# Attention and two MLPs in one kernel: value blocks as long rows, other orders for the first weights, turns ahead of local scores

## What is computed

```python
q_d = q.reshape(B, H, Sd, 4, D).mean(axis=3)          # the same for k_d, v_d; Sd = 144
out_up = np.repeat(sm_attn(q_d, k_d, v_d), 4, axis=2)
mask = np.abs(pos[:, None] - pos[None, :]) < 4
scores = np.where(mask, scale * np.matmul(q, k.transpose(0, 1, 3, 2)), -1e9)
attn = softmax(scores)
x = (out_up + np.matmul(attn, v))                      # as (2304 tokens, 512)
h = x @ w_in;  x = (h - np.tanh(h)) @ w_out            # d_ff 2048
gate = 1.0 / (1.0 + np.exp(-(x @ w_gate)))
out = (gate * (x @ w_val)) @ w_out2                    # d_ff 1536
```

## Time and profile before

| | us |
|---|---|
| median of 3 runs (lowest, highest) | 932.12 (931.35, 934.47) |
| profiled execution, its own time | 935.37 |
| span of the profile | 933.6 |
| mean granted clock of TensorE | 0.982 |

### The profile page before, as it was taken

The page is one execution under the profiler, slowest core; times in us unless marked ns, Lnnn a source line. Parts: engine busy times, 40 slices in busy tenths (PEclk is TensorE's granted clock), DMA queues, the critical chain, the costliest instruction groups (busy, mean ns, idle before and its releaser), DMA issues.

```text
span 933.6 us, 15654 instructions
## 1 busy us (share of the span) xinstructions
PE 894.9 (96%) x6056; PEld 837.6 (90%) x6056; DVE 588.9 (63%) x919; ACT 387.2 (41%) x752; POOL 294.0 (31%) x237
## 2 busy tenths in 40 slices
PE   7889987999999999999998999999999999999997
PEld 4666786999999999999997999999999999999996
DVE  7778884757865657765668556566544456544444
ACT  5667953435432325332343644454222233222221
POOL 5789946773103000020016565722200001000000
PEclk9798998999999999999999999999999999999999
DMA  8989837667564545454421777769775555565511
GB/s 234 208 182 221 229 121 296 251 242 296 195 217 157 217 156 211 160 213 157 170 91 46 284 292 280 280 281 368 280 285 206 211 205 204 205 269 203 203 45 68
DMA packets 46089, 197.01 MB, mean 211 GB/s; under 512 B 3936, under 2 KB 15552, under 8 KB 33216
## 3 DMA queue, kind: packets, MB, share of 16 engines
q1 hardware_dynamic: 41984, 166.66, 51.4%
q0 software_dynamic: 4032, 29.36, 8.3%
HBM read 139.90 MB, written 56.10 MB: 210 GB/s over the span
## 4 chain that ended last, share of the span: by engine, by line
PE 83%; DMA 4%; DVE 3%; ACT 3%; POOL 3%; issue 3%; SPq 1%; ACTq 0%; DVEq 0%
PE banks L827 43%; PE banks L899 19%; PE banks L1016 16%; DMA v_win<-in_v_dram 2%; DMA win_raw<-in_moe_w_in_dram 1%; PE banks L805 1%; DVE x_op L1368 1%; PE banks L782 1%; DMA qk<-in_k_dram 1%; ACT prob_d L1058 1%; POOL win L619 1%; POOL mid L633 1%; ACT win L1080 1%; PE banks L818 1%; PE banks L760 1%
## 5 line engine op out<-in xcount | busy, mean ns | idle before, releaser
L827 PE MATMUL banks<-x_op,pair 128*128 128x384 f32 x1512 | 276.9, 335 | 1.8 <-DVE cg_sum L1545 1.8
L827 PEld LDWEIGHTS banks<-x_op,pair 128*128 128x128 f32 x1512 | 265.2, 188 | 9.7 <-DVE cg_sum L1545 2.1
L899 PE MATMUL banks<-g_parts,mid 128*128 128x384 f32 x1152 | 228.2, 337 | 12.8 <-DVE x_all L1447 6.7
L899 PEld LDWEIGHTS banks<-g_parts,mid 128*128 128x128 f32 x1152 | 203.6, 189 | 14.7 <-DVE x_all L1450 7.7
L827 PE MATMUL banks<-x_op,win 128*128 128x384 f32 x1008 | 203.7, 337 | 2.7 <-ACT x_op L1117 1.4
L827 PEld LDWEIGHTS banks<-x_op,win 128*128 128x128 f32 x1008 | 178.3, 189 | 4.0 <-ACT x_op L1117 1.9
L1016 PE MATMUL banks<-wout,p_parts 128*128 128x512 f32 x648 | 163.6, 393 | 1.7 <-issue 1.7
L1450 DVE TENSOR_TENSOR x_all<-banks,x_all 128x384 f32<-128x384 f32 x168 | 92.6, 555 | 78.2 <-PE banks L899 77.7
L1016 PEld LDWEIGHTS banks<-wout,p_parts 128*128 128x128 f32 x648 | 120.2, 188 | 22.6 <-issue 2.1
L1570 DVE TENSOR_TENSOR x_all<-banks,x_all 128x512 f32<-128x512 f32 x90 | 62.1, 690 | 113.3 <-PE banks L1016 113.3
L1138 ACT ACTIVATE banks<-c_sum 128x384 f32<-128x384 f32 x72 | 35.2, 489 | 96.9 <-DVE c_sum L1417 52.6
(11 more groups left out here) (97 smaller groups left out, 1009.0 us busy)
## 6 DMA issues: line engine op xcount, KB each, us to landing
pair<-kept_pair SPq DMA_DIRECT2D x24, 1792.0 KB, 10.8
win<-kept_in SPq DMA_DIRECT2D x16, 1792.0 KB, 7.3
kept_pair<-pair SPq DMA_DIRECT2D x12, 1792.0 KB, 12.0
mid<-kept_mid POOLq DMA_DIRECT2D x16, 1024.0 KB, 5.1
kept_in<-win SPq DMA_DIRECT2D x7, 1792.0 KB, 5.8
wout<-kept_out POOLq DMA_DIRECT2D x12, 1024.0 KB, 11.6
kept_mid<-mid SPq DMA_DIRECT2D x7, 1024.0 KB, 6.2
kept_out<-wout SPq DMA_DIRECT2D x6, 1024.0 KB, 14.9
```

What stands on the lines that cost most here:

```text
L827: mm = pe.matmul(bk[:, 0:T], weights[:, w, p - 1, kk, :], x_op[:, p - 1, x, kk, :], start=(first and kk == 0 and a == 0), stop=(last and k ...
L899: mm = pe.matmul(bk[:, 0:T], w[:, wp, f, m * P:(m + 1) * P], g[:, gp, 2 * f + t, :], start=(f == 0 and a == 0), stop=(f == 1 and a == 2))
```

## The change

1. The host writes a second copy of the values, `v_windows`, of shape (4, 4, 70, 9, 128): the 9 windows of a unit side by side, so that each of the 70 partitions of `v_win` is one contiguous row of 1152 elements, 4608 bytes. `load_v` is one DMA in place of three.
2. TensorE does the two `turn_local(t-1)` ahead of `local_scores(t+1)`.
3. Quad 2: its raw load at unit 8 (was 14), its sums in iterations 14 and 15 (were after the loop), its high part at iteration 17 (was after the copies of step 1).
4. From quad 3 on: the raw load of quad 3 stands ahead of the wait for the end of the attention; the sums on GpSimd are made one step earlier in the order (n+3, ahead of `plain_low(n+1)`), the low part after it; the high part of quad n+1 stands in step n ahead of tanh of C11 (was quad n+2, ahead of tanh of C21).
5. `x_high(0, 2)` moves from iteration 16 to the end of 15, and VectorE does `x_low(0, 4)` ahead of `second_weight_low`.

```diff
 def load_v(u):
     wait(sp, s_val, u - 1)
-    for w, n in ((0, 1), (1, NW - 2), (NW - 1, 1)):
-        src = bass.AP(unit.tensor, unit.offset + FIRST_KEY[w] * P, [[P, KW], [QW * P, n], [1, P]])
-        sp.dma_start(v_win[u % 2][:, w:w + n, :], src).then_inc(s_v[u % 2], 16)
+    sp.dma_start(v_win[u % 2][:, :, :], v_windows[u // PAIRS, u % PAIRS]).then_inc(s_v[u % 2], 16)
...
-                if u == 14:
+                if u == 8:
                     load_raw(2)
             load_raw_mid(1)
+            load_raw(3)
+            keep_win(1)
             sp.wait_ge(s_x, UNITS)
-            for n in range(N1):
-                if 3 <= n + 2 < Q1:
+            for n in range(1, N1):
+                if 4 <= n + 2 < Q1:
                     load_raw(n + 2)
                 elif Q1 <= n + 2 < N1:
                     load_win(n + 2)
-                if 1 <= n + 1 < Q1:
+                if n + 1 < Q1:
+                    load_raw_mid(n + 1)
                     keep_win(n + 1)
-                if 1 <= n < Q1:
+                if n < Q1:
                     keep_mid(n)
-                if 2 <= n + 1 < Q1:
-                    load_raw_mid(n + 1)
...
 GpSimd
-            weight_sums(2, (0, 1))
+                if t == 14:
+                    weight_sums(2, (0, 1))
+                if t == 15:
+                    weight_sums(2, (2, 3))
             x_last_sum(0)
-            weight_sums(2, (2, 3))
             weight_low(2)
             for n in range(N1):
-                if 3 <= n + 2 < Q1:
-                    weight_sums(n + 2)
-                    weight_low(n + 2)
+                if n + 3 < Q1:
+                    weight_sums(n + 3)
                 if n + 1 < Q1:
                     plain_low(n + 1)
+                if n + 3 < Q1:
+                    weight_low(n + 3)
                 if n % Q1 == 3:
                     x_sums(n // Q1 + 1)
...
 TensorE
-                if t + 1 < UNITS:
-                    local_scores(t + 1)
                 if 1 <= t <= UNITS:
                     turn_local(t - 1, 0)
                     turn_local(t - 1, 1)
                 if t + 1 < UNITS:
+                    local_scores(t + 1)
                     down_scores(t + 1)
...
 ScalarE, step n
+                if 3 <= n + 1 < Q1:
+                    weight_high(n + 1)
                 tanh(n, C11)
                 tanh(n, C22)
                 g_high(n, 0)
-                if 3 <= n + 2 < Q1:
-                    weight_high(n + 2)
 ScalarE, iteration t
                 if t == UNITS:
                     copy_c(0, C11)
-                    x_high(0, 2)
                     x_high(0, 5)
                 if t == UNITS + 1:
                     x_high(0, 4)
+                    act.wait_ge(s_vd, UNITS)
+                    weight_high(2)
                     tanh(0, C11)
...
+                if t == UNITS - 1:
+                    x_high(0, 2)
...
             copy_c(1, C21)
-            act.wait_ge(s_vd, UNITS)
-            weight_high(2)
             plain_high(1)
 VectorE, after the loop
+            x_low(0, 4)
             second_weight_low()
-            x_low(0, 4)
             add_c(0, C11)
```

More of the change, by code:

```diff
@@ L40, in attention_and_mlps @@
     v: bass.AP,
+    v_windows: bass.AP,
     w_in: bass.AP,
@@ L389, in load_v @@
             def load_v(u):
-                unit = v_flat[u * P * S:(u + 1) * P * S]
                 wait(sp, s_val, u - 1)
-                for w, n in ((0, 1), (1, NW - 2), (NW - 1, 1)):
-                    src = bass.AP(unit.tensor, unit.offset + FIRST_KEY[w] * P, [[P, KW], [QW * P, n], [1, P]])
-                    sp.dma_start(v_win[u % 2][:, w:w + n, :], src).then_inc(s_v[u % 2], 16)
+                sp.dma_start(v_win[u % 2][:, :, :], v_windows[u // PAIRS, u % PAIRS]).then_inc(s_v[u % 2], 16)
             def two_chunks(src, first, step):
@@ L798, in local_values @@
             def local_values(u):
-                pe.wait_ge(s_v[u % 2], 48 * (u // 2 + 1))
+                pe.wait_ge(s_v[u % 2], 16 * (u // 2 + 1))
                 pe.wait_ge(s_cl, 2 * (u + 1))
@@ L1642 @@
         args.append(nc.dram_tensor(f"in_{name}_dram", a.shape, _mybir.dt.from_np(a.dtype), kind="ExternalInput").ap())
+        if name == "v":
+            first = [min(max(64 * w - 3, 0), s - 70) for w in range(s // 64)]
+            a = _np.ascontiguousarray(_np.stack([a[:, :, f:f + 70, :] for f in first], axis=3))
+            arrays["in_v_windows_dram"] = a
+            args.append(nc.dram_tensor("in_v_windows_dram", a.shape, _mybir.dt.from_np(a.dtype), kind="ExternalInput").ap())
     shape = (b * s, h * d)
```

## The result

The changed kernel takes 921.84 us, the median of 4 runs (920.45 to 924.27), beside 933.3 for the kernel before in the same set (931.35 to 934.83): a ratio of 0.988, 95% interval 0.985 to 0.991. Two later sets of six gave medians of 923.25 and 921.96; over all 16 runs it is 922.0 (920.3 to 927.95). So the change gains 1.2%, where 909.0 us (904 to 920), 2.5%, was predicted. The profiled execution took 924.27 (span 922.5) against 935.37 (933.6), so 11.1 us have to be found where the sum said 23.1.

The account below looks back on a forecast made before the run. TensorE was 96% busy, with all that can move before 212 us: GpSimd's work and waits in the attention, VectorE's end, stalls in steps 2 and 5. 8.7 + 2.8 + 12.6 - 1.0 = 23.1 off 932.12 gave 909.0 us, range 904 to 920.

Parts of the forecast that it names:

- Step 1: Attention's value blocks as 4608 B rows: 3.0 us less queue time per unit, GpSimd's early waits 11.6 us shorter.
- Rival A: Short rows were no burden, so the attention's early waits stay: 920.6 us, 8%.
- Step 2: Turns ahead of local scores on TensorE in the attention: counted 0, bounds -1 and +1 us.
- Step 3: Quad 2's sums inside GpSimd's full attention loop: costs 2.9 us; its high part costs 0.
- Step 5: End of the attention, from `normalise(15)` to product 3 of step 0: 11.6 us in place of 14.4, gain 2.8.
- rival B: GpSimd's low part of quad 2 goes first and VectorE waits 4.1 us at the attention's end: 913.1 us, 20%.
- Step 4: Quads 3 on in the first MLP: TensorE's stalls in steps 2 and 5, 8.9 and 3.7 us, both go: 12.6.
- Quad 7: Its sums come late behind `x_sums(1)` in step 6: 1.0 us lost, bounds 0 and 3.7.
- Rival C: In the new order of quads 3 to 7 one stall remains or comes, priced 8.9 us: 917.9 us, 10%.
- Rival D: Turns bind VectorE to GpSimd within one attention unit, 2.9 us lost in each of 14: 950 us, 5%.

Follow-up runs that it names:

- experiment 2: Kernel before with only the host's value layout and one DMA in place of three: 933.0 us, ratio 1.001 to the kernel before.
- the bench: Loads alone, without attention and MLPs, 12 blocks of each kind: 70 partitions took 21.1 us with 512 B rows, 20.1 with 4608 B; 128 rows of 2520 B 13.2.
- experiment 5: Changed kernel with both value blocks of a unit written over 128 partitions from unit 2 on (values then wrong): 915.94 us, ratio 0.983 to the kernel before.
- experiment 4: Changed kernel with local scores put ahead of the turns again: 924.21 us, ratio 0.992 to the kernel before.
- Experiment 8: Changed kernel with quad 2's four weight sums put back behind the last attention unit: 921.6 us, ratio 0.989 to the kernel before.
- experiment 10: Kernel before with only the new order of loads, sums and splits for the late quads: 924.1 us, ratio 0.992 to the kernel before.
- experiment 6: Changed kernel with the first middle weights loaded after unit 5's value block, not unit 2's: 922.26 us, ratio 0.988 to the kernel before.
- experiment 13: Changed kernel with quad 2's sums behind the last unit and quad 7's middle weights ahead of the first reload: 921.25 us, ratio 0.991 to the kernel before.

## Why the prediction was wrong

**Step 1 failed, and makes up nearly all of the miss:** 11.6 us were counted and experiment 2 shows none, of the 12.8 between 909.0 and 921.84. It put 0.100 us on each 512 B packet because 2494 of them stood in a stretch with a full queue. The other packets there were priced at the rate of a stretch with only 128-partition transfers, and the whole rest was charged to the short ones. But the groups cover 72 partitions and were slow too, and the long rows cover 70 and stayed slow. A block went from 21.1/12 = 1.8 us to 1.7 in the bench, not from 3.9 to 0.9. The term that was mis-sized is the 0.100 us per packet: in the bench's stretch of 70 short rows, 17 us x 16 engines x 0.99 over the 6840 packets that 206 GB/s make, it is about 0.039 us. The packets under 2 KB did fall as was said, from 15552 to 5024 in the whole profile, and nothing came of it. With experiment 5 the waits did go, so what comes next, GpSimd at its own pace, was right as well. The Trainium skill states what decides, on the page "SBUF — State Buffer", section "Door 1: The DMA port swizzle (why `[64,N]` ≈ `[32,N]`)": partitions 0 to 63 reach half of the ports and 64 to 127 the other half, while a step of 32 stays on the same port. The rows agree: 64 rows at 0 (208 GB/s) as slow as 32 rows (208), and 64 rows at 32 (343) nearly as fast as 128 (365). The page that the prediction weighed, "DMA: Bandwidth & Descriptors" of the Trainium skill, section "Specifications", has 512 B as the smallest transfer for line rate; here that held to within 5 to 8% (206 against 217 GB/s over 70 partitions, 334 against 360 over 128). Rival A's premise, that short rows are no burden, thus held, at 8%, and its time, 920.6, is the nearest of all.

**Step 2** was counted as nothing; experiment 4 resolves no difference (924.21 us against 921.84 to 923.25).

**Step 3** was priced at 2.9 us; the two classes of profiles lie 62 and 65 us apart from N5 to N15, so some 3.5. With step 1 at nothing, N15 should move from 113.5 to 117; it was 109.5 to 115.0 in three executions, whose waits up to N5 differ by 6.6 us.

**Step 5** said +2.8, and N15 to F became 2.3 shorter; that the size came out right is in part luck, for step 5's own order is not what did it. Experiment 8 keeps that order, puts only the sums back behind the loop, and N15 to F is 20.1 again. The working had VectorE "no longer alternating with GpSimd" there, which is step 3's doing: the gain hangs on the sums, and what step 5 adds to it no run shows. VectorE came first, as chosen, and `second_weight_low` took 2.02, so rival B did not come; ScalarE's x_high of 4 kept VectorE waiting 4.71 us, which the working had as a series without a gap. GpSimd's low part took 5.19 us in place of 4.08; it started 1.27 us before `second_weight_low` ended, and lies off the path.

**Step 4** was right: 12.6 predicted, 12.7 measured, and shown to stand alone by experiment 10. The high part cost nothing in its gap, as said.

**Quad 7** was taken as 1.0 us lost with a bound of 3.7; it is 2.5, and by another way. The sums were in time (ScalarE's high part at 207.43 waited for nothing). What was called hidden by 1 us, `plain_low(5)` with its block behind it, was only followed to its store; behind the store in SyncE's queue stood a reload of 1.8 MB and then the middle weights.

**Rival C** is that gap, at 2.5 us and not 8.9. **Rival D** did not come: N5 to N15 grew by 3.5 us, not by ten times 2.9.

## What to carry to other kernels

Before a transfer's rows are made longer, look at which partitions it covers: blocks of 64 or 70 partitions from partition 0 got 200 to 230 GB/s with rows of 512 and of 4608 bytes alike, where 128 partitions got 330 to 365, and 64 that begin at partition 32 got 343. When a mixed, full queue is to be priced, take the prices from transfers of the same shape and not as a rest. On an engine without gaps, work moved to start earlier costs its whole length there, and the end it was moved from must gain more than that: here 3.5 us were paid for 2.3. Where a new order moves a store, follow SyncE's queue behind it to the next load that somebody waits for.

## What was not expected of the hardware

The executions of one and the same kernel differ by up to 10 us, and the mean granted clock goes with it: one kernel (experiment 6) took 928.15 us at a clock of 0.982 and 918.13 at 0.992, and over all runs of all kernels, each kernel with a level of its own, 0.01 of mean clock goes with 5 us. It does not hold run by run: of the first four executions of the changed kernel the slowest, 924.27 us, had the highest clock, 0.993. The profiles put it in the attention: each of the two MLPs behind differs by some 2 us at most, N15 by 6.8 (109.5 to 116.3 over four profiles with the same attention). One stretch of low clock there, 38 to 45 us in the changed kernel at 0.57, begins where TensorE had waited 2.95 us for a value block. Whether the clock lengthens the attention or only follows its waits is not settled: no run held the one and varied the other. At equal clock, by that fit, experiment 13 would be 2.4 us ahead of the changed kernel and the changed kernel 1.3 ahead of experiment 10, which is a fit and no measurement.
